# Attention and two mixture layers in one kernel: the stretch between the last expert and the first sorted tile rewritten

## The chip, the cores and the metric

The kernel runs on one core of a Trainium2 chip. The metric is the device time of one execution in microseconds; a lower number is better. TensorE (PE) multiplies, with its weight loads apart (PEld); VectorE (DVE), ScalarE (ACT) and GpSimd (POOL) do elementwise work; SyncE (SP) issues most transfers, and POOL those whose rows are chosen by an index in memory.

## What is computed

The reference is a chain of three stages. The first is attention with hashed buckets; its result, 1536 tokens of 512 numbers, goes through an expert layer in which every expert sees every token, and then through one in which each token goes to one expert:

```python
out = np.zeros((N, D))                       # second stage, N, D, E, F = 1536, 512, 8, 1024
for e in range(E):
    out += P[:, e:e + 1] * (np.maximum(x @ w1[e], 0.0) @ w2[e])
# third stage, on x = out
xn = x / (np.linalg.norm(x, axis=-1, keepdims=True) + 1e-06)
logits = xn @ en.T / tau                     # en: normalised expert_emb
expert_idx = np.argmax(logits, axis=1)
probs = softmax(logits)                      # exp(logits - max) / (sum + 1e-9)
gate_w = probs[np.arange(N), expert_idx]
for e in range(E):
    mask = expert_idx == e
    out[mask] = gate_w[mask, None] * (np.maximum(x[mask] @ w1[e], 0.0) @ w2[e])
```

## The kernel before

Every product in single precision is made of three matmuls on split operands (`matmul_x3`, L444 to L446: low by high, high by high, high by low), so each weight matrix must be split into a high and a low part before use. ACT makes the high parts and DVE the low ones.

**The second stage** goes over 8 experts. An expert works in three groups of 512 tokens, each first up (8 blocks `f`) and then down (8 blocks for 4 token tiles `i` of 128). After each down sum DVE adds the tile to `tok` (L1569). In the last expert, routing of the finished tiles is woven between the matmuls. A token tile `t` (0 to 11) passes these steps: PE turns it (`turn_token`, L793); ACT copies it out as `x_t` (L1091) and takes its sum of squares; PE makes the logits (`token_logits`, L799); DVE chooses the expert (`choose`, L1433 to L1439); PE ranks the tokens (`token_rank`, L804, L805); DVE finds each token's cell (`find_cell`, L1446 to L1463); and PE adds the tile to a table of cells (`table_part`, L811).

**Between the stages** stands the stretch that the change rewrites. Tile 11 is ready only with the very last sum, and passes its steps with nothing beside it. The first sorted tile consists of rows gathered from `x_rows` in memory, where tiles 0 to 9 are stored (an index list, `first_idx`, L1483, a gather by POOL, L585 with `x_row`, and a product with a diagonal matrix `diag`, L939), plus rows of tiles 10 and 11 that are taken from `tok` with a one-hot matrix `hot` (`last_rows`, L838). `HOT` is 10. The sum lies in PSUM banks 2 to 5. ACT and DVE split it into `x_hi` (L1169) and `x_lo` (L1628). Meanwhile DVE makes the inverse norms and the softmax weights of all tokens (L1606 to L1612, with an Exp on ACT at L1197, then L1639 to L1641), and PE and DVE the starts of the experts' tiles (L949, L950, `start_i` at L1618) and the list of rows (L956, L1632 to L1635).

**The third stage** runs over sorted tiles of 128 rows, each with one expert. Each engine goes over the experts' tiles in loops whose bounds it loads from `start_i` (L450, L451). Beside a tile, ACT and DVE split the next expert's weights (L1115 and L1503 for `w2`, L1110 and L1497 for `w1`), and ACT scales the tile before and puts it into `y_row` (L1175), for which it needs the weights `p_now`. POOL's order for a tile is: copy the indices, store `y_row`, gather `p_now` from `weights`, gather the rows of the tile after next. It begins when DVE's weights (`p_ready`) have been stored to memory by SP. SP loads the experts' weights, 2 MB each, in the order written out, as the buffers come free; the load for `w1` of expert 2 waits for the weights' store and for the second gather of rows.

What waits on what is fixed by semaphores and by the order of the code on each engine; nothing is planned at run time but the loop bounds.

## Time and profile before

| | us |
|---|---|
| median of 3 runs | 1612.83 (1612.45 to 1616.38) |
| the profiled execution | 1612.79 |
| its span | 1611.1 |
| PE busy | 1578.6 (98%) |
| DVE busy | 682.7 (42%) |
| ACT busy | 507.7 (32%) |
| POOL busy | 311.4 (19%) |
| granted clock of PE over the span | 0.99 |

The span is the profiled stretch of work; about 1.7 us of the execution's time lie around it. A busy share is an average over all three stages, and the change touches a stretch of about 18 us, so the shares tell little about it. A granted clock of 1.00 means 2.4 GHz, one of 0.50 means 1.2 GHz.

### The profile page before, as it was taken

The page shows a single profiled execution, that of the slowest core. Times are in us where ns is not written, and L with a number is a line of the kernel's source. Part 1 is how long each engine was busy: PE and PEld are TensorE (multiplying, and loading weights), DVE is VectorE, ACT ScalarE, POOL GpSimd, SP SyncE. Part 2 cuts the span into 40 slices and gives each one's busy share as a digit, 9 for nine tenths or more (in the row PEclk, how much of TensorE's full clock was granted, in tenths as well). Part 3 has the DMA queues.
Part 4 walks back from the last instruction along what each step waited for, and adds up shares of the span by engine and source line. Part 5 has one row for each costly group of instructions (what it writes and reads, how often), then busy time and mean ns, then how long its engine had stood idle before and what let it go on. Part 6 is the DMA issues. An engine that isn't in the chain of part 4 may idle for free.

```text
span 1611.1 us, 21916 instructions
## 1 busy us (share of the span) xinstructions
PE 1578.6 (98%) x7637; PEld 1318.6 (82%) x7638; DVE 682.7 (42%) x1237; ACT 507.7 (32%) x933; POOL 311.4 (19%) x522
## 2 busy tenths in 40 slices
PE   7999999999999999999999999999999999899997
PEld 6999998778888888888888888888888887778886
DVE  5888788351211211322221121122232255787666
ACT  4777777211100101211210111021121133476554
POOL 4455443200210120030030021003003000132222
PEclk8999999999999999999999999999999999799999
DMA  6554554100110110110020011011002121574310
GB/s 153 136 128 112 126 121 146 71 1 0 52 53 1 52 52 0 52 52 0 0 100 4 0 52 52 0 52 52 0 0 105 40 79 72 187 291 148 140 46 25
DMA packets 45592, 110.96 MB, mean 69 GB/s; under 512 B 5926, under 2 KB 7974, under 8 KB 45552
## 3 DMA queue, kind: packets, MB, share of 16 engines
q1 hardware_dynamic: 41248, 100.52, 20.1%
q0 software_dynamic: 3504, 8.14, 1.5%
q10 hardware_dynamic: 800, 1.77, 0.5%
q8 instruction: 24, 0.39, 0.1%
q14 instruction: 16, 0.13, 0.0%
HBM read 81.57 MB, written 8.39 MB: 56 GB/s over the span
## 4 chain that ended last, share of the span: by engine, by line
PE 90%; DVE 3%; issue 2%; POOL 2%; DMA 2%; ACT 1%; POOLq 0%; DVEq 0%; ACTq 0%
PE psum L444 25%; PE psum L446 25%; PE psum L445 25%; PE psum L682 3%; PE psum L671 2%; PE psum L695 2%; PE psum L696 1%; PE psum L672 1%; PE psum L653 1%; DVE row_min L1263 1%; PE psum L707 1%; PE psum L971 1%; DVE pt_lo L1253 1%; PE psum L799 1%; DMA x_row<-x_rows,idx_now 1%
## 5 line engine op out<-in xcount | busy, mean ns | idle before, releaser
L1123 ACT ACTIVATE h_hi<-psum 128x512 fp32r<-128x512 f32 x192 | 115.0, 599 | 890.5 <-PE psum L446 890.5
L444 PE MATMUL psum<-xt_lo,w_hi 128*128 128x512 f32 x768 | 305.5, 398 | 0.2 <-DVE xt_lo L1356 0.2
L446 PE MATMUL psum<-xt_hi,w_lo 128*128 128x512 f32 x768 | 304.5, 396 | 0.0
L445 PE MATMUL psum<-xt_hi,w_hi 128*128 128x512 f32 x768 | 304.4, 396 | 0.0
L444 PE MATMUL psum<-w_lo,h_hi 128*128 128x512 f32 x768 | 302.3, 394 | 0.0
L446 PE MATMUL psum<-w_hi,h_lo 128*128 128x512 f32 x768 | 299.3, 390 | 0.0
L445 PE MATMUL psum<-w_hi,h_hi 128*128 128x512 f32 x768 | 299.1, 389 | 0.0
L1514 DVE SCALAR_TENSOR_TENSOR h_lo<-psum,h_hi 128x512 fp32r<-128x512 f32 x192 | 132.8, 692 | 368.5 <-ACT h_hi L1123 368.5
L1569 DVE SCALAR_TENSOR_TENSOR tok<-psum,route,tok 128x512 f32<-128x512 f32 x84 | 57.5, 745 | 355.3 <-PE psum L446 355.3
L477 POOL CAST w_hi<-w_raw 128x512 fp32r<-128x512 f32 x64 | 40.0, 626 | 823.1 <-PE psum L446 813.8
L444 PEld LDWEIGHTS psum<-xt_lo,w_hi 128*128 128x128 f32 x768 | 144.6, 188 | 35.1 <-DVE xt_lo L1356 0.4
L446 PEld LDWEIGHTS psum<-xt_hi,w_lo 128*128 128x128 f32 x768 | 144.6, 188 | 35.1
L445 PEld LDWEIGHTS psum<-xt_hi,w_hi 128*128 128x128 f32 x768 | 144.7, 188 | 34.5
L446 PEld LDWEIGHTS psum<-w_hi,h_lo 128*128 128x128 f32 x768 | 144.1, 188 | 30.4
L444 PEld LDWEIGHTS psum<-w_lo,h_hi 128*128 128x128 f32 x768 | 144.2, 188 | 29.0
L445 PEld LDWEIGHTS psum<-w_hi,h_hi 128*128 128x128 f32 x768 | 144.3, 188 | 28.9
L1253 DVE TENSOR_TENSOR pt_lo<-psum,pt_hi 128x384 fp32r<-128x384 f32 x192 | 98.2, 553 | 35.8 <-ACT pt_hi L1020 34.0
L1027 ACT ACTIVATE prob<-psum,row_bias,row_scale 128x768 f32<-128x768 f32 x96 | 96.6, 1007 | 20.7 <-POOL row_bias L521 20.5
L1020 ACT CAST pt_hi<-psum 128x384 fp32r<-128x384 f32 x192 | 83.3, 487 | 42.4 <-PE psum L682 42.4
L1263 DVE TENSOR_REDUCE row_min<-psum 128x1 f32<-128x768 f32 x96 | 91.1, 949 | 8.7 <-PE psum L672 8.7
L560 POOL TENSOR_TENSOR w_lo<-w_raw,w_hi 128x512 fp32r<-128x512 f32 x64 | 82.7, 1291 | 12.4 <-issue 7.2
L671 PE MATMUL psum<-k_b,q_b 128*128 128x384 f32 x192 | 74.7, 389 | 7.6 <-DMA q_b<-bits 5.0
(264 smaller groups left out, 2026.8 us busy)
## 6 DMA issues: line engine op xcount, KB each, us to landing
w_raw<-in_moe_w_dram SPq DMA_DIRECT2D x25, 2048.0 KB, 8.2
w_raw_odd<-in_moe_w_dram SPq DMA_DIRECT2D x4, 2048.0 KB
k_hh<-k_hi SPq DMA_DIRECT2D x32, 192.0 KB, 3.0
w_raw_even<-in_moe_w_dram SPq DMA_DIRECT2D x3, 2048.0 KB
x_rows<-tok SPq DMA_DIRECT2D x14, 256.0 KB, 2.4
k_raw<-in_k_dram SPq DMA_DIRECT2D x8, 384.0 KB, 3.0
v_raw<-in_v_dram SPq DMA_DIRECT2D x16, 192.0 KB, 3.4
k_b<-k_lo SPq DMA_DIRECT2D x16, 192.0 KB, 3.4
```

What stands on the lines that cost most here:

```text
L444: pe.matmul(acc, a[0], b[1], start=start, stop=False)
L445: pe.matmul(acc, a[0], b[0], start=False, stop=False)
L446: return pe.matmul(acc, a[1], b[0], start=False, stop=stop)
L560: pool.tensor_tensor(w2_s[1][:, f, :], w2_raw[:, f, :], w2_s[0][:, f, :].bitcast(F32), ALU.subtract).then_inc(m1.w2_lo, 1)
L671: pe.matmul(o, q_b[u][:, a], k_b[u][:, b], start=True, stop=False)
L1020: act.copy(pt_hi[half][:, 3 * c:3 * c + 3, a:a + P], psum[:, 4 + c, 0:HALF].rearrange("p (j i) -> p j i", j=3)).then_inc((s_hi_a, s_hi_b)[ ...
L1027: act.activation(prob[t % 2][:].rearrange("p (c j) i -> p c (j i)", c=2), psum[:, 2 * (t % 2):2 * (t % 2) + 2, 0:HALF], ACT.Exp, bias=row_ ...
L1123: act.activation(h_s[0][:, f, :], psum[:, f % 4, :], ACT.Relu).then_inc(m1.h_hi, 1)
L1253: dve.tensor_tensor(pt_lo[half][:, 3 * c:3 * c + 3, a:a + P], psum[:, 4 + c, 0:HALF].rearrange("p (j i) -> p j i", j=3), pt_hi[half][:, 3 ...
L1263: dve.tensor_reduce(row_min[:, c], psum[:, 2 * (t % 2):2 * (t % 2) + 2, 0:HALF], AX.XY, ALU.min).then_inc(s_min, 1)
L1514: dve.scalar_tensor_tensor(h_s[1][:, f, :], psum[:, f % 4, :], 0.0, h_s[0][:, f, :].bitcast(F32), ALU.max, ALU.subtract).then_inc(m1.h_lo, 1)
L1569: dve.scalar_tensor_tensor(tok[:, tile, 0:DM], psum[:, 4 + i, :], route[:, e, tile:tile + 1], tok[:, tile, 0:DM], ALU.mult, ALU.add).then_ ...
```

## The change

Seven things change. (1) The last sum, that of tile 11, is made in two halves of 256 columns, and PE's turn and ACT's copy follow in halves (`turn_half`, `last_token`). (2) The list `first_idx` is asked for one block earlier (`f == 4` for 5), and DVE's split of the last part of `w1` (L1497) moves from before it to behind `choose(10)`. (3) The product with the gathered rows is parted: columns 0 and 1 of four stay ahead of tile 11's logits, 2 and 3 go behind tile 10's last table part, just ahead of tile 11's rows. (4) Inverse norms and softmax sums go from DVE to POOL, but for three reciprocals; the sum of eight is made by three adds. POOL does this between its first and its second gather. (5) ACT takes its Exp behind a wait for the tiles' starts. (6) PE turns the identity four times ahead of tile 11's logits and four times behind the last table part (`keep_busy`). (7) The loop over expert 0's tiles stands ahead of the others with start 0 and an end that ACT and DVE load earlier.

The core of the diff; new semaphores, and the same change of the loop (7) in DVE's part, are left out.

```diff
@@ -609,6 +611,28 @@
         pool.wait_ge(s_x_stored, 16 * HOT)
         pool.wait_ge(s_first_idx, 1)
         gather(x_row[:], x_rows, first_idx[:], s_xrow)
+        squares, inv = per_tok[:, 0, :], per_tok[:, 3, :]
+
+        def row_bc(i):
+            return per_tok[:, i, :].unsqueeze(2).to_broadcast([P, TT, E])
+
+        pool.wait_ge(s_total_in, 1)
+        pool.tensor_tensor(g1[:], logit[:], row_bc(4), ALU.subtract).then_inc(s_p_step, 1)
+        pool.wait_ge(s_norm, 1)
+        pool.tensor_tensor(inv, inv, squares, ALU.mult).then_inc(s_p_step, 1)
+        pool.wait_ge(s_p_step, 2)
+        pool.tensor_tensor(inv, inv, per_tok[:, 2, :], ALU.add).then_inc(s_p_step, 1)
+        pool.wait_ge(s_p_step, 3)
+        pool.tensor_scalar(inv, inv, 0.5, 1e-6, ALU.mult, ALU.add).then_inc(s_p_step, 1)
+        pool.wait_ge(s_norm, 2)
+        pool.tensor_tensor(g1[:], g1[:], row_bc(3), ALU.mult).then_inc(s_act_in, 1)
+        pool.wait_ge(s_act_out, 4)
+        for n in (4, 2):
+            pool.tensor_tensor(g1[:, :, 0:n], g1[:, :, 0:n], g1[:, :, n:2 * n], ALU.add).then_inc(s_p_step, 1)
+            pool.wait_ge(s_p_step, 4 + 4 // n)
+        pool.tensor_tensor(squares, g1[:, :, 0], g1[:, :, 1], ALU.add).then_inc(s_p_step, 1)
+        pool.wait_ge(s_p_step, 7)
+        pool.tensor_scalar(per_tok[:, 1, :], squares, 1e-9, None, ALU.add).then_inc(s_p_sum, 1)
         pool.wait_ge(m2.routed, 1)
         pool.wait_ge(s_x_last, 32)
         pool.wait_ge(s_xrow_t, 1)
@@ -836,14 +860,14 @@
             pe.wait_ge(s_hot, t - HOT + 1)
             for kd in range(KD):
                 mm = pe.matmul(psum[:, 2 + kd, 0:P], tok[:, t, kd * P:(kd + 1) * P], hot[:, t - HOT, :],
-                               start=False, stop=t == TT - 1)
+                               start=t == HOT and kd >= 2, stop=t == TT - 1)
             if t == TT - 1:
                 mm.then_inc(s_xrow_t, 1)
 
         def tokens_between(f, i, n):
 
             t = 2 * CT - 1 + i
-            if t == HOT and f == 5:
+            if t == HOT and f == 4:
                 pe.wait_ge(s_added, 3)
...
@@ -932,23 +956,48 @@
-        turn_token(TT - 1, 0)
-        pe.wait_ge(s_diag, 1)
-        pe.wait_ge(s_xrow, 16)
+
+        def keep_busy(n, bank):
+            for i in range(n):
+                pe.transpose(psum[:, bank, 0:P], ident[:], ident[:])
+
+        def gathered_rows(kds):
+            pe.wait_ge(s_diag, 1)
+            pe.wait_ge(s_xrow, 16)
+            for kd in kds:
+                pe.matmul(psum[:, 2 + kd, 0:P], x_row[:, kd * P:(kd + 1) * P], diag[:], start=kd < 2, stop=False)
+
+        def turn_half(half, bank):
+            for kd in (2 * half, 2 * half + 1):
+                a = kd % 2 * P
+                tr = pe.transpose(psum[:, bank, a:a + P], tok[:, TT - 1, kd * P:kd * P + P], ident[:])
+            return tr
+
+        pe.wait_ge(s_squares, TT - 1)
+        pe.wait_ge(s_tok_half, 1)
+        turn_half(0, 0).then_inc(s_turn_half, 1)
+        pe.wait_ge(m1.y, E * TT + 1)
+        turn_half(1, 7).then_inc(s_turned, 1)
+        gathered_rows((0, 1))
+        keep_busy(4, 5)
         for kd in range(KD):
-            pe.matmul(psum[:, 2 + kd, 0:P], x_row[:, kd * P:(kd + 1) * P], diag[:], start=True, stop=False)
-        token_logits(TT - 1, 1)
+            if kd % 2 == 0:
+                pe.wait_ge(s_copied, TT + kd // 2)
+            mm = pe.matmul(psum[:, 1, 0:E], x_t[:, kd, :], emb_t[:, kd, :], start=(kd == 0), stop=(kd == KD - 1))
+        mm.then_inc(s_logits, 1)
         last_rows(HOT)
         token_rank(TT - 1, 6)
         pe.wait_ge(s_total_in, 1)
         pe.matmul(psum[0:E, 1, 32:33], counts[:, TT % 2, :], ones_b[:, 0:1], start=True, stop=True).then_inc(s_total, 1)
         pe.wait_ge(s_squares, TT)
         table_part(HOT, 0)
+        gathered_rows((2, 3))
         last_rows(TT - 1)
         pe.wait_ge(s_begin_in, 1)
         pe.matmul(psum[0:CELLS, 6, 32:33], earlier[0:E, :], spot[0:E, 5:6], start=True, stop=True)
         pe.matmul(psum[0:1, 6, 48:48 + E + 1], spot[0:E, 4:5], reach[0:E, :], start=True, stop=True).then_inc(s_begin, 1)
         table_part(TT - 1, 0)
+        keep_busy(4, 7)
         pe.wait_ge(s_start, 1)
...
@@ -1091,6 +1140,17 @@
             act.wait_ge(s_copied, t + 1)
             act.activation(psum[:, bank, :], tok[:, t, :], ACT.Square,
+                           accum_out=per_tok[:, 0, t:t + 1]).then_inc(s_squares, 1)
+
+        def last_token():
+            t = TT - 1
+            act.wait_ge(s_logits, t)
+            act.wait_ge(s_turn_half, 1)
+            act.copy(x_t[:, 0:2, :].rearrange("p k i -> p (k i)"), psum[:, 0, 0:256]).then_inc(s_copied, 1)
+            act.wait_ge(s_turned, TT)
+            act.copy(x_t[:, 2:4, :].rearrange("p k i -> p (k i)"), psum[:, 7, 0:256]).then_inc(s_copied, 1)
+            act.wait_ge(s_copied, TT + 1)
+            act.activation(psum[:, 0, :], tok[:, t, :], ACT.Square,
                            accum_out=per_tok[:, 0, t:t + 1]).then_inc(s_squares, 1)
@@ -1193,15 +1252,17 @@
                 w1_hi2(e + 1, w1_raw_of[1 - u])
 
         first_x_hi()
+        act.wait_ge(s_start, 1)
+        first_end = act.value_load(start_i[0:1, 1:2], min_val=1, max_val=SLOTS)
         act.wait_ge(s_act_in, 4)
         act.activation(g1[:], g1[:], ACT.Exp).then_inc(s_act_out, 1)
-        act.wait_ge(s_start, 1)
         act.wait_ge(s_x_lo, 1)
+        tiles2(0, 0, 0, first_end)
         with act.Fori(0, E // 2 - 1) as e2:
-            for u in range(2):
-                expert2(2 * e2 + u, u)
-        expert2(E - 2, 0)
-        expert2(E - 1, 1, more=False)
+            for u in (1, 0):
+                e = 2 * e2 + 2 - u
+                tiles2(e, u, *tile_range(act, e))
+        tiles2(E - 1, 1, *tile_range(act, E - 1), more=False)
...
@@ -1450,6 +1511,8 @@
                                               chosen[:, 0:1].to_broadcast([P, P]), ALU.is_equal, ALU.mult))
                 dve.sem_inc(s_hot, 1)
             if t == TT - 1:
+                dve.wait_ge(s_act_out, 3)
+                dve.reciprocal(per_tok[:, 3, :], per_tok[:, 2, :]).then_inc(s_norm, 1)
                 dve.wait_ge(s_total, 1)
                 link(dve.tensor_scalar(spot[0:E, 6:7], psum[0:E, 1, 32:33], P / 2 - 0.5, EVEN, ALU.add, ALU.add))
                 link(dve.tensor_scalar(spot[0:E, 4:5], spot[0:E, 6:7], EVEN, float(P), ALU.subtract, ALU.max))
@@ -1561,16 +1624,24 @@
                         if i == 0:
                             w1_lo2(0, w1_raw, (0,))
                         choose(2 * CT - 1 + i, 1)
+                        if i == CT - 1:
+                            w1_lo2(0, w1_raw, (KD - 1,))
                         dve.wait_ge(*((s_down_tile, i + 1) if i < CT - 1 else (m1.down, n + 2)))
                     tile = c * CT + i
                     if first:
                         first_y(tile)
                         continue
+                    if last and tile == TT - 1:
+                        for half, done in ((slice(0, 256), s_tok_half), (slice(256, 512), m1.y)):
+                            dve.scalar_tensor_tensor(tok[:, tile, half], psum[:, 4 + i, half], route[:, e, tile:tile + 1],
+                                                     tok[:, tile, half], ALU.mult, ALU.add).then_inc(done, 1)
+                        find_cell(HOT, 6)
+                        continue
                     dve.scalar_tensor_tensor(tok[:, tile, 0:DM], psum[:, 4 + i, :], route[:, e, tile:tile + 1],
                                              tok[:, tile, 0:DM], ALU.mult, ALU.add).then_inc(m1.y, 1)
                     if last and c == CH - 1:
-                        find_cell(2 * CT - 1 + i, 6 if i == CT - 1 else 2)
-                        if i < CT - 1:
+                        find_cell(2 * CT - 1 + i, 2)
+                        if i < CT - 2:
                             w1_lo2(0, w1_raw, (i + 1,))
                         if i == 2:
                             add_part(HOT - 1, 3)
@@ -1601,16 +1672,9 @@
-        dve.wait_ge(s_act_out, 3)
-        root, inv = per_tok[:, 2, :], per_tok[:, 3, :]
-        link(dve.reciprocal(inv, root))
-        link(dve.tensor_tensor(inv, inv, per_tok[:, 0, :], ALU.mult))
-        link(dve.tensor_tensor(inv, inv, root, ALU.add))
-        link(dve.tensor_scalar(inv, inv, 0.5, 1e-6, ALU.mult, ALU.add))
-        link(dve.reciprocal(inv, inv))
-        link(dve.tensor_tensor(g1[:], logit[:], row_bc(4), ALU.subtract))
-        link(dve.tensor_tensor(g1[:], g1[:], row_bc(3), ALU.mult))
-        dve.sem_inc(s_act_in, 1)
+        inv = per_tok[:, 3, :]
+        dve.wait_ge(s_p_step, 4)
+        dve.reciprocal(inv, inv).then_inc(s_norm, 1)
         dve.wait_ge(s_begin, 1)
         link(dve.tensor_copy(begin_col[0:CELLS, :], psum[0:CELLS, 6, 32:33]))
         link(dve.tensor_scalar(slot_of[0:CELLS, :], slot0[0:CELLS, :], begin_col[0:CELLS, 0:1], None, ALU.is_equal))
@@ -1635,9 +1699,8 @@
         link(dve.scalar_tensor_tensor(tab[:, 1:COLS, 0:1], out_at[:, 0:COLS - 1].unsqueeze(2), -1.0,
                                       ids[:, 0:COLS - 1].unsqueeze(2), ALU.add, ALU.add))
         dve.sem_inc(m2.routed, 1)
-        dve.wait_ge(s_act_out, 4)
-        link(dve.tensor_reduce(per_tok[:, 0, :], g1[:], AX.X, ALU.add))
-        link(dve.tensor_scalar(per_tok[:, 1, :], per_tok[:, 0, :], 1e-9, None, ALU.add))
+        first_end = dve.value_load(start_i[0:1, 1:2], min_val=1, max_val=SLOTS)
+        dve.wait_ge(s_p_sum, 1)
         link(dve.reciprocal(per_tok[:, 2, :], per_tok[:, 1, :]))
         dve.sem_inc(s_p_ready, 1)
 
```

**PE from tile 11's turn on.** `tok` turned is L793 before and L973 now; L799 and L986 are the logits of tile 11, L939 and L968 the gathered rows, L838 and L862 the rows of tile 10. Before:

```order
L793 MATMUL psum<-ident,tok 128x128 [waits token_squares,m1_y_added]
L793 MATMUL psum<-ident,tok 128x128 x3
L939 MATMUL psum<-diag,x_row 128x128 [waits x_row_loaded,diag_ready]
L939 MATMUL psum<-diag,x_row 128x128 x3
L799 MATMUL psum<-emb_t,x_t 128x8 [waits token_copied]
L799 MATMUL psum<-emb_t,x_t 128x8 x3
L838 MATMUL psum<-hot,tok 128x128 [waits last_rows_one_hot]
L838 MATMUL psum<-hot,tok 128x128 x3
L804 MATMUL psum<-chosen,prior 128x8 [waits token_chosen]
```

And now:

```order
L973 MATMUL psum<-ident,tok 128x128 [waits last_sum_half,token_squares]
L973 MATMUL psum<-ident,tok 128x128
L973 MATMUL psum<-ident,tok 128x128 [waits m1_y_added]
L973 MATMUL psum<-ident,tok 128x128
L968 MATMUL psum<-diag,x_row 128x128 [waits x_row_loaded,diag_ready]
L968 MATMUL psum<-diag,x_row 128x128
L962 MATMUL psum<-ident 128x128 x4
L986 MATMUL psum<-emb_t,x_t 128x8 [waits token_copied]
L986 MATMUL psum<-emb_t,x_t 128x8
L986 MATMUL psum<-emb_t,x_t 128x8 [waits token_copied]
L986 MATMUL psum<-emb_t,x_t 128x8
L862 MATMUL psum<-hot,tok 128x128 [waits last_rows_one_hot]
```

The turn waits for halves, two of the gathered rows' columns are gone from ahead of the logits, and four turns of the identity stand there.

**PE from tile 10's table part to the first sorted tile.** L811 and L835 are the table part, L949 and L997 the starts, L956 and L1005 the list of rows. Before:

```order
L811 MATMUL psum<-lane_id,cell 96x128 [waits table_added,token_cell,token_squares]
L838 MATMUL psum<-hot,tok 128x128 [waits last_rows_one_hot]
L838 MATMUL psum<-hot,tok 128x128 x3
L949 MATMUL psum<-spot,earlier 96x1 [waits begins_wanted]
L950 MATMUL psum<-reach,spot 1x9
L811 MATMUL psum<-lane_id,cell 96x128 [waits token_cell]
L953 TENSOR_LOAD start_i [waits starts_ready]
L953 ISA x2
L956 MATMUL psum<-slot_of,table 128x21 [waits slots_wanted,table_added]
```

And now:

```order
L835 MATMUL psum<-lane_id,cell 96x128 [waits table_added,token_cell,token_squares]
L968 MATMUL psum<-diag,x_row 128x128 [waits x_row_loaded,diag_ready]
L968 MATMUL psum<-diag,x_row 128x128
L862 MATMUL psum<-hot,tok 128x128 [waits last_rows_one_hot]
L862 MATMUL psum<-hot,tok 128x128 x3
L997 MATMUL psum<-spot,earlier 96x1 [waits begins_wanted]
L998 MATMUL psum<-reach,spot 1x9
L835 MATMUL psum<-lane_id,cell 96x128 [waits token_cell]
L962 MATMUL psum<-ident 128x128 x4
L1002 TENSOR_LOAD start_i [waits starts_ready]
L1002 ISA x2
L1005 MATMUL psum<-slot_of,table 128x21 [waits slots_wanted,table_added]
```

Two columns of the gathered rows now stand between tile 10's table part and tile 11's rows, and four turns of the identity ahead of the load of a bound.

**POOL between its first gather and its loops.** Before:

```order
L585 DMA x_row<-x_rows,first_idx 128x512 [waits first_idx_ready,x_stored]
L585 DMA x_row<-x_rows,tab 128x512 [waits x_row_turned,x_last_stored,m2_routed]
L617 UNCONDITIONAL_BRANCH [waits p_stored]
```

And now:

```order
L587 DMA x_row<-x_rows,first_idx 128x512 [waits first_idx_ready,x_stored]
L620 TENSOR_TENSOR g_61<-logit,per_tok 128x96 [waits totals_wanted]
L622 TENSOR_TENSOR per_tok<-per_tok 128x12 [waits norm_inverse]
L624 TENSOR_TENSOR per_tok<-per_tok 128x12 [waits p_step_pool]
L626 TENSOR_SCALAR per_tok<-per_tok 128x12 [waits p_step_pool]
L628 TENSOR_TENSOR g_61<-g_61,per_tok 128x96 [waits norm_inverse]
L631 TENSOR_TENSOR g_61<-g_61 128x12x4 [waits route_act_out]
L631 TENSOR_TENSOR g_61<-g_61 128x12x2 [waits p_step_pool]
L633 TENSOR_TENSOR per_tok<-g_61 128x12 [waits p_step_pool]
L635 TENSOR_SCALAR per_tok<-per_tok 128x12 [waits p_step_pool]
L587 DMA x_row<-x_rows,tab 128x512 [waits x_row_turned,x_last_stored,m2_routed]
L641 UNCONDITIONAL_BRANCH [waits p_stored]
```

Nine elementwise instructions, each with a wait, stand ahead of the second gather.

## Rows read from the trace of the kernel before

**Rows 1.** Stages: us, busy us of PE, PEld, DVE, ACT, POOL; PEclk, DMA share, GB/s

```profile
1371.00:1376.00 5.00, 3.27 (x16) 1.94 (x16) 3.26 (x15) 0.23 (x1) 1.30 (x1) 0.99 0.22 68
1376.00:1382.00 6.00, 5.93 (x28) 5.68 (x28) 2.60 (x15) 1.29 (x4) 0.00 (x0) 0.50 0.99 289
1382.00:1389.00 7.00, 3.97 (x17) 3.44 (x17) 5.10 (x22) 2.15 (x3) 0.00 (x0) 0.50 0.21 80
1400.00:1410.00 10.00, 10.00 (x48) 8.04 (x48) 9.96 (x14) 8.46 (x14) 2.12 (x3) 1.00 0.85 278
```

**Rows 2.** Timeline of PE, from the last expert to the first sorted tile

```profile
1373.08 0.18 PE L804 MATMUL psum<-chosen,prior 128*128 128x8 bf16 x1 [0.49 <-DVEq L1437]
...
1375.02 0.66 PE L793 MATMUL psum<-ident,tok 128*128 128x128 f32 x4 [0.92 <-DVE tok L1569]
1376.07 2.04 PE L939 MATMUL psum<-diag,x_row 128*128 128x128 f32 x8 [0.40 <-DMA x_row<-x_rows,first_idx]
1377.91 1.71 PE L799 MATMUL psum<-emb_t,x_t 128*128 128x8 f32 x8
1379.48 2.05 PE L838 MATMUL psum<-hot,tok 128*128 128x128 f32 x8
...
1382.46 2.08 PE L838 MATMUL psum<-hot,tok 128*128 128x128 f32 x8 [0.45 <-DVEq L1451]
...
1388.00 0.58 PE L956 MATMUL psum<-slot_of,table 96*128 96x21 f32 x2 [2.58 <-DVEq L1477]
```

**Rows 3.** Timeline of DVE in the same stretch

```profile
1368.39 1.23 DVE L1497 TENSOR_TENSOR w_lo<-w_raw,w_hi 128x1024 fp32r<-128x1024 f32 x1
...
1371.14 0.16 DVE L1483 TENSOR_SCALAR first_idx<-psum 128x1 uint32<-128x1 f32 x1 [1.33 <-PE psum L848]
...
1374.21 0.75 DVE L1569 SCALAR_TENSOR_TENSOR tok<-psum,route,tok 128x512 f32<-128x512 f32 x1 [0.73 <-PE psum L446]
...
1379.66 0.17 DVE L1433 TENSOR_REDUCE per_tok<-psum 128x1 f32<-128x8 f32 x1 [2.39 <-PE psum L799]
...
1381.60 0.17 DVE L1446 TENSOR_TENSOR pick<-psum,chosen 128x8 f32<-128x8 f32 x1 [0.22 <-PE psum L805]
...
1384.38 0.23 DVE L1606 RECIPROCAL per_tok<-per_tok 128x12 f32<-128x12 f32 x1
...
1386.21 0.15 DVE L1615 COPY begin_col<-psum 96x1 f32<-96x1 f32 x1
...
1386.78 0.15 DVE L1618 TENSOR_SCALAR start_i<-psum 1x9 int32<-1x9 f32 x1
```

**Rows 4.** Timeline of ACT, its table load, Exp and two rows of output

```profile
1385.18 1.28 ACT L1197 ACT_TABLE_LOAD   x1
1386.47 0.28 ACT L1197 ACTIVATE g<-g 128x96 f32<-128x96 f32 x1
...
1390.38 0.69 ACT L1175 ACTIVATE y_row<-psum,p_now 128x512 f32<-128x512 f32 x1 [3.62 <-issue]
...
1417.12 0.69 ACT L1175 ACTIVATE y_row<-psum,p_now 128x512 f32<-128x512 f32 x1 [1.86 <-POOLq L607]
```

**Rows 5.** Chain that ended last, pieces by start and length

```profile
1372.28 3.65 DMA x_row<-x_rows,first_idx
...
1390.10 0.24 DVE per_tok L1641
...
1399.86 8.12 DMA x_row<-x_rows,idx_now
```

**Rows 6.** Groups by line and shape, the nearest POOL operation

```profile
L511 POOL TENSOR_TENSOR v_s<-v_raw,v_s 128x384 fp32r<-128x384 f32 x16 | 16.1, 1009 | 1.4
```

**Rows 7.** Timeline of PE at the start of the program

```profile
3.38 4.67 PE L634 MATMUL psum<-ident 128*128 128x128 f32 x24
...
8.07 0.33 PE L653 MATMUL psum<-k_hi,proj_k_lo 128*128 128x384 f32 x1
...
16.32 0.52 PE L672 MATMUL psum<-k_hh,q_t 128*128 128x384 f32 x1
```

More of the change, by code:

```diff
@@ L235, in program @@
     s_p_stored, s_p = sem("p_stored"), sem("p_loaded")
+    s_tok_half, s_turn_half = sem("last_sum_half"), sem("last_turn_half")
+    s_norm, s_p_step, s_p_sum = sem("norm_inverse"), sem("p_step_pool"), sem("p_sum_ready")
     s_diag, s_hot, s_start = sem("diag_ready"), sem("last_rows_one_hot"), sem("starts_ready")
@@ L1147, in expert @@
                     token(2 * CT + 2, 0)
-                    token(2 * CT + 3, 0)
+                    last_token()
             if not last:
@@ L1175, in y_tile, with tiles2 @@
             act.activation(y_row[:], psum[:, 4, :], ACT.Copy, scale=p_now[:, 0:1]).then_inc(s_y2, 1)
-        def expert2(e, u, more=True):
-            first, end = tile_range(act, e)
+        def tiles2(e, u, first, end, more=True):
             with act.Fori(first, end) as i:
@@ L1652, in g_lo, with tiles2 @@
                               ALU.subtract).then_inc(s_g_lo, 1)
-        def expert2(e, u, more=True):
-            first, end = tile_range(dve, e)
+        def tiles2(e, u, first, end, more=True):
             with dve.Fori(first, end) as i:
@@ L1674, in expert2 @@
                 w1_lo2(e + 1, w1_raw_of[1 - u])
+        tiles2(0, 0, 0, first_end)
         with dve.Fori(0, E // 2 - 1) as e2:
-            for u in range(2):
-                expert2(2 * e2 + u, u)
-        expert2(E - 2, 0)
-        expert2(E - 1, 1, more=False)
+            for u in (1, 0):
+                e = 2 * e2 + 2 - u
+                tiles2(e, u, *tile_range(dve, e))
+        tiles2(E - 1, 1, *tile_range(dve, E - 1), more=False)
     block.__exit__(None, None, None)
```

## The prediction

> **What bounds the kernel now.** The table of the profile came first: the profiled execution took 1612.79 us, its span is 1611.1 us and PE is busy for 98% of it. So PE sets the time nearly everywhere, and the change can only bring what PE loses in its stretch. I then read the stages between the last expert and the first sorted tile [rows 1]. In three of them PE has less than its full time, 3.27 of 5.00, 5.93 of 6.00 and 3.97 of 7.00 us, and in two the granted clock is 0.50, which is 1.2 GHz. The 0.99 of the first shows that the clock fell at its very end.
>
> The timelines tell what the path is. PE waits 0.49 us for tile 10's choice, 0.92 us for the last sum and 0.40 us for the first gather [rows 2], which left at 1372.28 and took 3.65 us [rows 5]. Tile 11's logits then stand behind the gathered rows, 1376.07 to 1377.91, and last to 1379.48. Its rank stands behind tile 10's rows, so that DVE picks it up at 1381.60 [rows 2, 3]. I call this moment R. From there DVE is the path: cell, norms and softmax weights, starts. `start_i` is written at 1386.93 (1386.78 and 0.15), which I call T [rows 3]. PE loads a bound, makes the list of rows at 1388.00 and begins the first sorted tile about 0.45 us later, at T + 1.5 [rows 2].
>
> Behind T a second path matters. DVE's weights are ready at 1390.34, T + 3.4; their store and POOL's order for a tile follow, with a gather of rows that takes 8.12 us to land [rows 5], for the 3.65 of the calm one. At 1417.12 ACT had waited 1.86 us for POOL before it could scale a tile [rows 4]. DVE is busy 9.96 of 10.00 us from 1400 to 1410 [rows 1]. So up to the third tile four things are near their limit, and a head start of PE must be matched by POOL and DVE to reach the end.
>
> **The change, part by part.** I make each sum twice: A with the clock at 0.50 from about 1376 as before, B with it at 1.00 as far as T.
>
> *Up to the logits.* `first_idx` is asked for a block earlier and no longer stands behind the split of 1.23 us [rows 3]. An estimate is 1.4 us, by which the first gather lands near 1374.5. Tile 10's choice moves as well, so PE's wait of 0.49 us goes and the last sum starts at 1373.7 for 1374.21. The moved split then lies beside PE's last twelve matmuls or so, and ends about when the last sum can begin; if that cover is gone, it costs up to 1.2 us. Half a sum of 0.75 us, 512 columns, should take between 0.38 and 0.75; I take 0.48, since short operations on DVE cost 0.15 alone [rows 3]. The second turn ends near 1375.1, and the copy of each half lies beside what follows on PE. Then PE does four passes of gathered rows. They cost 0.25 us each at 0.50 (2.04 for eight, [rows 2]) and an estimated 0.13 at 1.00. Four turns of the identity come behind them, 0.19 each (4.67 for 24, [rows 7]) at 0.50, and about half at 1.00. Logits begin at 1376.9 in A and at 1375.9 in B, for 1377.91 before.
>
> *Up to R.* In A the rest is as long as before: R comes 1.0 us earlier. In B the logits take 0.8 for 1.57 us (gain 0.8). Tile 10's rows take half of 2.0, but then tile 11's choice, some 0.95 us on DVE from 1379.66 [rows 3], is what the rank waits for (gain 0.6). R comes 2.0 + 0.8 + 0.6 = 3.4 us earlier.
>
> *From R to T*, 5.33 us before. DVE loses the 1.83 us from 1384.38 to 1386.21 [rows 3] and keeps two reciprocals of 0.23 with their links, so it could take the starts at R + 3.2 for R + 4.6. POOL's chain of three small operations between the reciprocals hides behind DVE's cell. But PE has to deliver the starts, and has four passes of gathered rows more ahead of tile 11's rows. In A these are 1.0 us, half of which the wait of 0.45 us for `hot` covers [rows 2]; the starts come at R + 3.9. In B they come at R + 2.4, and DVE sets R + 3.2. With 0.7 us more for the starts, R to T is 4.6 in A and 3.9 in B. **T comes 1.0 + 0.7 = 1.7 us earlier in A and 3.4 + 1.4 = 4.8 us in B.** The second four turns (0.75 us in A) end before DVE has written T or just behind, and cost nothing up to some 0.4 us. The way from T to the first tile stays 1.5 us.
>
> *What the moved weights cost.* Before, the table load of 1.28 us and the Exp lay ahead of T on ACT [rows 4]. Now ACT first waits for T and loads a bound. Before, two loads and a wait of some 1.3 us for the first tile's low part made up the 3.62 us without work ahead of 1390.38 [rows 4], so one load is about 0.9 (an estimate; between nothing and 1.8). Load, table, Exp: 0.1 + 0.9 + 1.28 + 0.28 = 2.6 us. Then come four operations on POOL of 48 elements and fewer. No row has this shape; 384 elements take 1.009 us [rows 6], which bounds each from above, and nothing is the bound below; I take 0.25 (nearer to the starts' 0.15 on DVE), 0.1 for each wait, 1.4 in all, and then 0.35 for DVE's reciprocal. Weights are ready at T + 4.4 for T + 3.4: **1.0 us of the head start is lost for POOL's path**, with up to 3.0 more at the upper bound. The second gather of rows, which was sent right behind the list, now waits for POOL's sums too, about T + 4.1 for T + 2.9; it lands at T + 7.7, still ahead of PE's turn of it at T + 9.7 (before, 8.2 us after a tile's start), or at T + 8.6 in B.
>
> Exp began right at the load's end, 1386.47 [rows 4], so I count no time between. The Trainium skill, ScalarE: Activation LUTs, "What ACT_TABLE_LOAD costs", gives 1283 ns for the load and some 1380 ns of draining on top. The trace agrees with the first and shows no second; by the page the weights would be 1.4 us later still.
>
> *What the transfers do.* A gather landed in 3.65 us in calm and in 8.12 us beside the 2 MB loads [rows 5]. POOL's gathers fall 1.0 us later relative to DVE, whose progress sends these loads, so they queue behind more of them. Bounds are a gain of 4.5 us (the calm case) and a loss of as much; I take a loss of 0.6. ACT's wait of 1.86 us shows that POOL's path is already on the edge, so this loss passes to PE. DVE enters its loop at T + 4.7 for about T + 5.5 (its weights and two loads), which leaves it 0.8 us in hand and costs nothing.
>
> **Sum.** Gain 1.7 to 4.8 at T, less 1.6. The clock fell after a spell in which PE waited 0.49, 0.92 and 0.40 us. Of these the first goes, the third goes, and four turns are added; it will fall, but later. I take the middle, 3.3 us, and get 3.3 - 1.6 = 1.7 us: 1612.8 - 1.7 = **1611.1 us**. The profiled execution's 1612.79 is the median's 1612.83 but for 0.04, so the sum needs no shift. The loops' new form costs a branch or two that no row shows, bounded by nothing below and by one load's 0.9 above; it is in the 0.9 that ACT saves in its loop's entry.
>
> **Rivals.**
>
> *The clock falls as before* (A). For it: four turns are 0.75 us at most in a stretch of 10, and PE is still without work for some 2 us ahead of the first tile. Against it: the waits before 1376 are 0.9 us shorter and work fills in. Then 1.7 - 1.6 leaves 0.1: 1612.7 us. Turning the identity does raise the clock in this kernel: after 24 turns and hardly anything else, a matmul of 384 columns takes 0.33 us at 8.07, and 0.52 at 16.32 behind a pause [rows 7], so the first ran at the full clock. The Trainium skill, TensorE: Matmul & The Clock Gate, "Part 4: PE-mode transpose", says that transposes don't count as activity for the clock; by it this rival would be certain, and the start of this trace speaks against it. I give it 0.25, my forecast 0.37.
>
> *The clock stays high to T, with the toll as reckoned*: 4.8 - 1.6 = 3.2, 1609.6 us, chance 0.12.
>
> *The clock stays high and the transfers fall well.* If the gather gets ahead of a 2 MB load, it gives back up to 4.5 us and POOL's path is free. Then DVE limits: 4.8 + 0.8 = 5.6, 1607.2 us. For it speaks that the order of gather and load is a matter of a microsecond; against it that POOL is moved to the wrong side. Chance 0.20.
>
> *POOL's path takes over*: its sums hold back the weights and the second gather, and with it SP's load for expert 2, which waits for both. At the upper price (3.0 more) and the full delay of a gather (4.5 for 0.6), the toll is 1.6 + 3.0 + 3.9 = 8.5, and with A's gain of 1.7 the kernel takes 1619.6 us. It turns slower by 0.3% when the toll passes the gain by 4.8, so at 6.5 in A. Against it speaks that nothing on POOL of this size took more than about a third of the upper price. Chance 0.06.
>
> **Numbers.** A measurement of this kernel can tell about 0.3%, 4.8 us, from no change, so the bounds are 1608.0 and 1617.6. Faster: 0.20, the free case. Slower: 0.06. The rest is within. The range goes down to the free case, 1607.0, and up to A with the sums at 0.5 us each on POOL (1.0 more) and a further 0.8 us for the gather, 1614.5; outside are the slower case and a tail of each.
>
> **What would show it.** In the profile after: PE's wait before the last choice gone; logits' start at 1376 to 1377; R at 1378 to 1381; T at 1382 to 1385.3; weights ready at T + 4.4; POOL's nine operations at 0.2 to 0.4 us each; a clock that falls after 1376; ACT's wait for POOL at the third tile longer than 1.86 us. The prediction would be wrong if the clock didn't fall at all, if the gathers land much faster or slower than 8 us, or if PE had slack behind the third tile, which its 98% don't show.

## The result, and the profile after

The changed kernel takes 1616.38 us (median; 1613.83 to 1618.30) and the kernel before, in turns with it on the same chips, 1612.37 (1610.27 to 1617.29). The ratio is 1.0017, with a 95% interval of 1.0010 to 1.0024. So the change costs 2.7 us by the ratio and 4.0 by the medians: less than the 0.3% that the prediction calls "no change", but the forecast was a gain, 1611.1, and its range ended at 1614.5. The profiled execution took 1614.12 us, its span is 1612.4 (1611.1 before). It is one of the 7 shorter of 22 executions (up to 1615.44; the other 15 took 1616.06 to 1618.30), so its trace shows only 1.3 us of the loss.

The way to the first sorted tile did get shorter. These are rows of DVE's timeline of the kernel after, which answer to [rows 3]:

```profile
1369.03 0.16 DVE L1546 TENSOR_SCALAR first_idx<-psum 128x1 uint32<-128x1 f32 x1 [0.58 <-PE psum L872]
...
1371.39 1.23 DVE L1560 TENSOR_TENSOR w_lo<-w_raw,w_hi 128x1024 fp32r<-128x1024 f32 x1
1372.95 0.87 DVE L1636 SCALAR_TENSOR_TENSOR tok<-psum,route,tok 128x256 f32<-128x256 f32 x2 [0.33 <-PE psum L448]
...
1378.35 0.17 DVE L1507 TENSOR_TENSOR pick<-psum,chosen 128x8 f32<-128x8 f32 x1
...
1382.08 0.16 DVE L1682 TENSOR_SCALAR start_i<-psum 1x9 int32<-1x9 f32 x1
```

and rows of PE's timeline, which answer to [rows 2]:

```profile
1375.04 0.96 PE L986 MATMUL psum<-emb_t,x_t 128*128 128x8 f32 x8
...
1377.48 0.18 PE L828 MATMUL psum<-chosen,prior 128*128 128x8 bf16 x1 [0.49 <-DVEq L1498]
...
1383.35 0.37 PE L1005 MATMUL psum<-slot_of,table 96*128 96x21 f32 x2 [1.39 <-DVEq L1540]
1383.76 0.71 PE L446 MATMUL psum<-w_lo,x_hi 128*128 128x512 f32 x1
```

The reader is to see R at 1378.35 (1381.60 before), T at 1382.24 (1386.93 before), and the first sorted tile at 1383.76, T + 1.5 as before. The start is 4.7 us earlier, nearly the 4.8 of case B. Of these, 0.3 are not the change's: ACT's last activation of the second stage, far ahead of the stretch, starts at 1343.36 and started at 1343.67 before.

Some 25 us later all of it is lost. POOL's timeline after:

```profile
1386.05 0.28 POOL L635 TENSOR_SCALAR per_tok<-per_tok 128x12 f32<-128x12 f32 x1
1386.77 1.04 POOL L587 DMA_INDIRECT x_row<-x_rows,tab  x1 [0.45 <-issue]
1390.81 0.19 POOL L479 COPY idx_now<-tab 128x3 uint32 x1 [2.99 <-DMA x_row<-x_rows,tab]
1396.11 1.24 POOL L596 DMA_INDIRECT out_dram<-y_row,idx_now  x1 [5.12 <-issue]
1397.65 1.92 POOL L587 DMA_INDIRECT p_now<-weights,idx_now  x1 [0.31 <-issue]
1399.88 0.95 POOL L587 DMA_INDIRECT x_row<-x_rows,idx_now  x1 [0.30 <-issue]
1407.64 0.19 POOL L479 COPY idx_now<-tab 128x3 uint32 x1 [6.81 <-DMA x_row<-x_rows,idx_now]
```

The same copy of the indices and the same three transfers in POOL's timeline before:

```profile
1395.54 0.69 POOL L477 COPY idx_now<-tab 128x3 uint32 x1 [4.79 <-issue]
1397.24 1.03 POOL L594 DMA_INDIRECT out_dram<-y_row,idx_now  x1 [1.01 <-POOL idx_now L477]
1398.58 0.97 POOL L585 DMA_INDIRECT p_now<-weights,idx_now  x1 [0.31 <-issue]
1399.86 1.47 POOL L585 DMA_INDIRECT x_row<-x_rows,idx_now  x1 [0.30 <-issue]
```

POOL had its indices at 1391.00, 5.2 us earlier than before (1396.23), and stored its first tile only 1.1 us earlier. In front of that store stand 5.12 us in which it waited for nothing that the profile shows ("issue"), for 1.01 before. What queues up behind it shows in ACT's timeline and in the list of PE's waits from 1383 to the end (us in total, times, longest), both after:

```profile
1404.67 0.69 ACT L1235 ACTIVATE y_row<-psum,p_now 128x512 f32<-128x512 f32 x1 [7.10 <-POOLq L609]
```

```profile
PE psum L1020 <- DVE g_row L1709: 5.6, 1, 5.6
PE psum L1005 <- DVEq L1540: 1.4, 1, 1.4
```

ACT lacks the weights' row `p_now` for 7.10 us (1.86 at 1417.12 in [rows 4], a tile later), DVE waits for ACT, PE lacks `g_row` for 5.6 us. And the stages after, in 4 us each, show a second price (columns as in [rows 1]):

```profile
1380.00:1384.00 4.00, 2.11 (x16) 1.59 (x15) 2.97 (x12) 1.17 (x2) 0.60 (x3) 0.98 0.46 173
1384.00:1388.00 4.00, 4.00 (x12) 3.10 (x12) 1.82 (x6) 3.99 (x8) 2.05 (x5) 0.60 0.05 4
...
1404.00:1408.00 4.00, 0.16 (x1) 0.16 (x2) 2.11 (x4) 3.33 (x7) 0.19 (x1) 0.54 1.01 375
1408.00:1412.00 4.00, 4.00 (x16) 3.35 (x17) 2.85 (x5) 2.21 (x5) 2.05 (x2) 0.61 0.52 210
```

PE works 0.16 of 4.00 us, and the granted clock falls to 1.2 GHz again. From 1408 to 1412 it is 0.61 in the mean, which is 0.39 x 4.00 = 1.6 us of work lost.

**What POOL waited for.** The DMA view counts one more kind of packet: "q14 instruction". From 1393 to 1395, after:

```profile
q1 hardware_dynamic: 201, 0.82, 103.0%
q14 instruction: 1, 0.01, 1.0%
```

One packet of 8 KB is fetched from a queue named for instructions, in the midst of SP's 2 MB load for expert 2, which left at 1390.56. Narrower windows put it at 1394.1; POOL's store follows 2.0 us later. Such packets stand in every trace, so what matters is which of them moves. Before has them at 1371.0, 1389.3, 1405.8 and 1407.8 in this stretch, after at 1369.7, 1384.1, 1394.1 and 1408.9. The ones at 1389.3 and 1384.1 come some 2 us behind T in either kernel and are a pair; the one at 1394.1 has moved up from 1405.8 or 1407.8, where POOL was waiting for its gather anyway (6.89 us, until 1408.22). My theory after the result, **F**: the packet is a piece of POOL's own program; the change adds 9 operations and as many waits to POOL's stream and so moves the place at which the next piece is needed; it is now needed when the rings are full of a 2 MB load, and POOL stands still. Its rivals: the **late gather**, that is the toll of the moved sums (the second gather of rows and the weights come too late), and **chance** in how transfers meet.

### The profile page after: what moved, and what is told of

Same layout as the page of the kernel before. It is cut to its first block, busy times and chain, and to the rows that moved or that the text cites. A ratio compares the mean times of both kernels' runs of the same rounds, so it can differ in the third digit from the quotient of the medians.

```text
span 1612.4 us, 21929 instructions
## 1 busy us (share of the span) xinstructions
PE 1576.7 (98%) x7645; PEld 1316.7 (82%) x7646; DVE 680.9 (42%) x1231; ACT 507.8 (31%) x934; POOL 312.7 (19%) x531
## 4 chain that ended last, share of the span: by engine, by line
PE 91%; DVE 3%; issue 2%; POOL 2%; DMA 1%; ACT 1%; DVEq 0%; POOLq 0%; ACTq 0%
PE psum L446 26%; PE psum L448 25%; PE psum L447 25%; PE psum L706 3%; PE psum L695 2%; PE psum L719 2%; PE psum L720 1%; PE psum L696 1%; PE psum L677 1%; DVE row_min L1324 1%; PE psum L731 1%; PE psum L1020 1%; DVE pt_lo L1314 1%; PE psum L823 1%; PE psum L770 0%
## 5 line engine op out<-in xcount | busy, mean ns | idle before, releaser
L706 PE MATMUL psum<-ident,prob 128*128 128x128 f32 x576 | 80.0, 274 | 1.0 <-DVE pt_lo L1314 0.8
```

Of the source, the lines that this page charges most:

```text
L706: tr = pe.transpose(psum[:, 4 + c, j * P:j * P + P], prob[par][:, 3 * c + j, :], ident[:])
```

## The experiments

**1. After, with 24 more instructions on POOL.** They repeat a table at the start of the program (once per instruction, with a wait behind each), almost 1400 us ahead of the place in dispute. No work of the kernel is touched.

```diff
+        for n in range(24):
+            pool.iota(slot_i[:], [[P, COLS]], base=0, channel_multiplier=-P).then_inc(s_pad, 1)
+            pool.wait_ge(s_pad, n + 1)
         pool.iota(slot_i[:], [[P, COLS]], base=0, channel_multiplier=-P).then_inc(s_pool_step, 1)
```

> The changed kernel, with 24 tiny index operations (iota) more on POOL, which repeat the last of its tables while POOL has nothing to do, far ahead of its first gather. Nothing on any path changes but the place of POOL's later instructions in its code. Theory F (a stretch of POOL's code is fetched behind the 2 MB load, and POOL stands still for it at its first output store): the fetch comes 24 instructions earlier, in calm, the 5.1 us ahead of the store shrink to about 1, POOL's gathers go out ahead of the next loads, and the time is 1608 to 1610.5. Theory Q (POOL's path is late by its sums and the Exp behind the starts, and the gathers queue behind the loads whatever the code does): no difference, 1616.

Measured: 1609.08 us (1606.96 to 1612.67), ratio to before 0.9979 (0.9969 to 0.9989). POOL's timeline of this kernel:

```profile
1390.67 0.18 POOL L480 COPY idx_now<-tab 128x3 uint32 x1 [3.04 <-DMA x_row<-x_rows,tab]
1391.87 1.04 POOL L600 DMA_INDIRECT out_dram<-y_row,idx_now  x1 [1.02 <-issue]
1393.21 1.00 POOL L591 DMA_INDIRECT p_now<-weights,idx_now  x1 [0.30 <-issue]
1394.51 1.44 POOL L591 DMA_INDIRECT x_row<-x_rows,idx_now  x1 [0.30 <-issue]
```

The indices are ready as after (1390.85), and the load of 2 MB left as after, at 1390.42; but the store follows the copy of the indices by 1.02 us. The DMA view has no instruction packet from 1388 to 1402, and one at 1370.9 that after does not have. All three transfers have been begun before SP sends its next load at 1395.24. PE's waits from 1383 on:

```profile
PE psum L1009 <- DVEq L1544: 1.4, 1, 1.4
```

The wait of 5.6 us is gone, and 24 instructions more make the kernel 7.3 us faster, as F had it (1608 to 1610.5). POOL's sums and its second gather, at 1386.58, are where they were, so the late gather can't be the cause.

**2. Before, with 9 more.** The edit is the same with `range(9)`, on the kernel before: as many as the change adds.

> The kernel before, with 9 such index operations more on POOL, as many instructions as the change added there. Theory F: the same place of POOL's code is fetched behind the load as in the changed kernel, a stand of 3 to 5 us before the first output store appears, and the time is 1614 to 1618. Theory Q: no difference from before, 1612.4.

Measured: 1621.13 us (1618.49 to 1621.84), ratio 1.0055 (1.0041 to 1.0069). Its POOL timeline and, from 1398 to 1400, its DMA view:

```profile
1395.11 0.47 POOL L478 COPY idx_now<-tab 128x3 uint32 x1 [5.02 <-issue]
1400.82 1.03 POOL L598 DMA_INDIRECT out_dram<-y_row,idx_now  x1 [5.24 <-issue]
1402.16 1.91 POOL L589 DMA_INDIRECT p_now<-weights,idx_now  x1 [0.31 <-issue]
```

```profile
q14 instruction: 1, 0.01, 1.0%
```

Nine instructions of no use, at the start of POOL's program, cost this kernel 9 us at its 1400th: the same stand of 5.2 us at the same store, with the packet at 1398.8, 2.0 us ahead of it. PE waits 5.1 us for `g_row`. F had the mechanism, but the loss is larger than expected (1614 to 1618), and this trace, of 1618.49 us, shows some 6 of the 9 us.

**3. After, with the second gather ahead of POOL's four sums.** If the late gather is the cause, this should help.

```diff
+        pool.wait_ge(m2.routed, 1)
+        pool.wait_ge(s_x_last, 32)
+        pool.wait_ge(s_xrow_t, 1)
+        gather(x_row[:], x_rows, tab[:, 1, 1:2], s_xrow)
         pool.wait_ge(s_act_out, 4)
...
-        pool.wait_ge(m2.routed, 1)
-        pool.wait_ge(s_x_last, 32)
-        pool.wait_ge(s_xrow_t, 1)
-        gather(x_row[:], x_rows, tab[:, 1, 1:2], s_xrow)
```

> The changed kernel with the second gather of rows put ahead of POOL's four sums. Theory F: the count of instructions ahead of the first output store is the same, the stand stays or grows, since the 2 MB load behind this gather starts earlier; 1615 to 1618. Theory Q: this gather and what hangs on it come some 1 to 2 us earlier, 1613 to 1615.

Measured: 1619.05 us (1618.94 to 1620.26), ratio 1.0043 (1.0028 to 1.0058). POOL's timeline:

```profile
1391.85 0.19 POOL L479 COPY idx_now<-tab 128x3 uint32 x1 [4.15 <-issue]
1398.07 3.65 POOL L596 DMA_INDIRECT out_dram<-y_row,idx_now  x1 [6.03 <-issue]
```

The gather leaves at 1385.40 (1386.77 after), but so does SP's load, 1388.88 for 1390.56, and the instruction packet comes at 1396.0. The stand grows to 6.0 us, the store's own issue takes 3.65, ACT waits 10.2 us. That is above both expectations, 1613 to 1615 and 1615 to 1618. It isn't a clean test of the late gather: with it, the weights' store falls back to 1388.04 (1386.67 after), and POOL's indices are ready 1.0 us later than after, not earlier. It fits F in that an earlier load ahead of the packet goes with a longer stand.

**4. After, with inverse norms and softmax weights back on DVE** (part 4 of the change undone: the 9 operations leave POOL, reduce and two adds return to DVE).

> The changed kernel with inverse norms and softmax weights back on DVE; POOL has none of its nine operations, and Exp stays behind the starts on ACT. Theory F: no stand at the first output store; the starts come 1.2 to 1.8 us later than in the changed kernel; 1609 to 1611. Theory Q: the weights are ready 0.5 us earlier relative to the starts and 1 us later in all; 1615 to 1617.

Measured: 1609.84 us (1608.67 to 1611.19), ratio 0.9984 (0.9975 to 0.9993). The store is at 1395.29 with 1.01 us ahead of it. POOL's stream is as long as before, and the stand is gone (F: 1609 to 1611). The packets are placed as before, at 1387.2, 1405.3 and 1407.1. This alone doesn't tell F from the late gather; with kernels 1 and 2 it does, since they keep every sum where it was.

**5 and 8. Kernel 1 without `keep_busy`, and kernel 1 with the last sum whole.** With the stand away, do two other parts of the change pay?

```diff
-        keep_busy(4, 5)
...
-        keep_busy(4, 7)
```

```diff
-                        for half, done in ((slice(0, 256), s_tok_half), (slice(256, 512), m1.y)):
-                            dve.scalar_tensor_tensor(tok[:, tile, half], psum[:, 4 + i, half], route[:, e, tile:tile + 1],
-                                                     tok[:, tile, half], ALU.mult, ALU.add).then_inc(done, 1)
+                        dve.scalar_tensor_tensor(tok[:, tile, 0:DM], psum[:, 4 + i, :], route[:, e, tile:tile + 1],
+                                                 tok[:, tile, 0:DM], ALU.mult, ALU.add).then_inc(m1.y, 1)
```

> The changed kernel with the 24 index operations of e1_after_24_more and without the eight turns of the identity. Theory F says nothing on them. If the turns hold the clock: it falls between 1376 and 1381, the starts come 1 to 3 us later than in e1, and the time is 1610 to 1612. If they don't count as activity: the clock falls at about 1384 as in e1, and the time is e1's 1609.1 or up to 0.7 less for the work left out.

> As e1_after_24_more, with the last sum made whole (one operation of 512 columns); PE's turn and ACT's copy are still in two parts. By my sum the first turn starts 0.3 us later and the whole path shifts by 0.2 to 0.4 us: 1609.3 to 1609.5, which can't be told from e1's 1609.1; DVE's operation takes 0.75 us for the 0.87 of the two halves.

Measured: 1608.38 us (1606.50 to 1609.66), ratio 0.9972 (0.9961 to 0.9983), and 1608.56 us (1607.82 to 1610.87), ratio 0.9978 (0.9967 to 0.9988). Kernel 1 has 0.9979. Neither part brings anything that can be measured; a whole sum was expected to cost 0.2 to 0.4 us, which these runs can't tell. Without the turns the clock is 1.00 to past 1384 as well:

```profile
1380.00:1384.00 4.00, 2.37 (x18) 1.79 (x17) 2.95 (x15) 0.72 (x2) 1.01 (x5) 1.00 0.90 339
1384.00:1388.00 4.00, 3.00 (x8) 2.45 (x9) 1.72 (x7) 2.94 (x5) 1.00 (x4) 0.67 0.01 2
```

**6. Kernel 1 with ACT's Exp ahead of its wait for the starts** (part 5 undone; `act.wait_ge(s_start, 1)` and the load of `first_end` go behind the Exp).

> As e1_after_24_more, with ACT's Exp ahead of its wait for the starts, as it was before the change. Theory F with the toll of my prediction (POOL's path 1.0 us late relative to the starts, since the table load of 1.28 us and a load of a bound lie behind them): weights and second gather come about 2 us earlier, and the time is 1607 to 1608.5. Theory Q in its weak form (with the fetch gone, POOL's path no longer sets anything): 1609.1 as e1.

Measured: 1608.71 us (1606.97 to 1615.32), ratio 0.9984 (0.9971 to 0.9996), just above the expected 1608.5, but in two groups, nine executions at 1607 to 1611 and three at 1615.2 to 1615.3. The profiled execution is of the second (1615.32). Its POOL and SP timelines:

```profile
1394.29 5.39 POOL L591 DMA_INDIRECT p_now<-weights,idx_now  x1 [0.30 <-issue]
```

```profile
1394.37 0.38 SPq L440 DMA_DIRECT2D w_raw<-in_moe_w_dram  x1
```

POOL begins its gather 0.08 us ahead of SP's 2 MB load and is held for 5.39 us, for 1.00 in kernel 1; PE waits 7.1 us. That is a second way to the same loss, with no instruction packet in it. What holds POOL there is not shown. That the load is sent at the same moment isn't enough: in the kernel after and in kernel 2 POOL's gather of rows begins within 0.01 us of a load of 2 MB (1399.88 and 1399.87; 1404.37 and 1404.38), and takes 0.95 us. The kernel before has executions of 1616 to 1618 now and then, whose profile I don't have; that they are of this kind is a guess.

**7. Before, with 33 more.** The control for kernel 1: is it the change that gains, or the 24?

> The kernel before with 33 index operations more on POOL: the 9 of e2_before_9_more and 24 more. Theory F: the fetch comes early, in calm, no stand at the output store, 1612.3 as before. If instead the operations themselves, not the place of the code, made e2 slow: 1621 or more.

Measured: 1611.93 us (1610.74 to 1616.87), ratio 0.9999 (0.9987 to 1.0011). The store at 1395.81 has 1.01 us ahead of it. One packet has gone from the stretch (left behind T are 1387.9 and 1406.5) and stands at 1243.3 instead, where POOL has nothing to do. Before was in a good place already, so more instructions bring it nothing, and kernel 1's gain over it is the change's.

**9 and 10. The best of these, and SP kept behind POOL.** Kernel 6 without `keep_busy`, where SP in addition waits for a semaphore before its load of expert 3's `w2`: for POOL's first store and gather of `p_now` to land (9, `s_y_free`), or for the third gather of rows (10, `s_xrow`). The edit of 10:

```diff
             sp.wait_ge(m2.w2_lo, KF * (split_until + 1))
+            if e == 3:
+                sp.wait_ge(s_xrow, 48)
```

> As e5_no_turns (24 index operations, no turns), with Exp ahead of the starts as in e6, and with SP's 2 MB load of w2 for expert 3 held back until POOL's first pair of store and gather of p_now has landed. e6 showed POOL's gather of p_now taking 5.39 us when this load was issued at the same moment, 0.08 us apart, in the runs at 1615. Theory F extended (POOL stands wherever its own small transfers or descriptors meet a 2 MB load): both the stand and the slow runs go, 1605.5 to 1608. Rival: holding the load back makes it late for ACT at the fourth tile, 1609 or more.

> As e9_load_after_weights_row, but the load waits until the gather of rows behind it has landed as well. If the gather then lands in about 4 us for 8, the load is sent at about 1397, 2 us later than in e1, and the time is 1605 to 1607.5; if the load becomes late, more than e9's.

Measured: 1608.35 us (1607.41 to 1609.08), ratio 0.9974 (0.9965 to 0.9983), and 1608.16 us (1607.45 to 1609.05), ratio 0.9976 (0.9966 to 0.9986). In kernel 9 the load leaves at 1397.12, and POOL's gather of `p_now` is short:

```profile
1394.33 1.00 POOL L593 DMA_INDIRECT p_now<-weights,idx_now  x1 [0.30 <-issue]
```

None of their 19 executions is in the late group of kernel 6 (3 of 12); since these kernels lack the turns as well, and the group is small, that the wait removed it is likely and not shown. Both are slower than expected (1605.5 to 1608 and 1605 to 1607.5). They beat both given kernels, by some 4 and 8 us; between them and kernels 1, 5 and 8 the runs tell nothing apart.

**11. After, unpadded, with SP's load for expert 2 held back.** The packet stays where the change put it, and the load is taken away from in front of it.

```diff
         sp.wait_ge(m2.w1_lo, KD)
+        sp.wait_ge(s_y_free, 2)
         sp.wait_ge(m2.w1_in, 32)
         sp.dma_start(w1_raw_of[0][:], m2.wa[2]).then_inc(m2.w1_in, 16)
```

> The changed kernel with its code as it is, and SP's first 2 MB load of the stage (w1 for expert 2) held back until POOL's first store and gather have landed. Theory F: the fetch is still needed at the same place, but has no load ahead of it; the 5.1 us ahead of the store shrink to 1 to 2.5, the next load is not delayed by more than 5 us, and the time is 1607 to 1611. If the stand of POOL has nothing to do with the load, it stays at about 5 us and the time at 1616 or more.

Measured: 1612.75 us (1610.82 to 1614.43), ratio 1.0005 (0.9997 to 1.0014). POOL's and SP's timelines:

```profile
1391.69 0.19 POOL L480 COPY idx_now<-tab 128x3 uint32 x1 [2.94 <-DMA x_row<-x_rows,tab]
1394.72 1.19 POOL L597 DMA_INDIRECT out_dram<-y_row,idx_now  x1 [2.85 <-issue]
1396.22 1.98 POOL L588 DMA_INDIRECT p_now<-weights,idx_now  x1 [0.30 <-issue]
```

```profile
1399.88 0.37 SPq L433 DMA_DIRECT2D w_raw<-in_moe_w_dram  x1
```

Now nothing large is in the rings, and the packet is at 1392.8, 0.9 us behind the copy of the indices (3.1 us behind it after). The stand is 2.85 us: 1.8 over the 1.02 of a kernel that needs no packet, where the load made it 4.1 over. So by these two traces the fetch alone costs 1.8 us and the queueing behind the load 2.3 more. This way 3.6 of the 7.3 us come back, less than expected (1607 to 1611, with a stand of 1 to 2.5). The rest I put down to a load that is now 9 us late: PE waits for `w_lo`, for rows and for `g_row` by 0.2 to 1.3 us at a time between 1404 and 1420, and the windows show it busy 2.74 of 4.00 us from 1404 on.

## Why the prediction was wrong

**Where it was right.** The steps up to the starts: PE's waits for tile 10's choice and for the first gather gone; R within its window (1378 to 1381); T at 1382.24 (1382 to 1385.3); T + 1.5 to the first tile. The moved weights: POOL's operations took 0.20 to 0.38 us each, and DVE's last reciprocal ended at 1386.59, T + 4.35, where T + 4.4 was forecast. Exp began at 1384.71, right at the end of the table load (1383.42 + 1.28); so the further 1.4 us by the Trainium skill, ScalarE: Activation LUTs, "What ACT_TABLE_LOAD costs", did not show here either. Two details missed: the logits began at 1375.04, a microsecond ahead of the sign given for them (1376 to 1377), since the last sum started at 1372.95 and not at 1373.7; and tile 11's rank, which case B had waiting for its choice, did so for 0.49 us at 1377.48, so the logits' lead was gone again at R.

**The gain at T: right mechanism, wrong size.** I took 3.3, the middle of 1.7 and 4.8, since "it will fall, but later". The clock fell only at the first sorted tile (windows above: 0.98 up to 1384), and T came 4.7 us earlier. The reason given for it, that turns of the identity help, is not borne out: without them (kernel 5) the time is the same. But single traces differ. Kernels 9 and 10, without turns too, have a granted clock of 0.50 all through 1380 to 1388, and kernel 2, with nothing of the change, has 1.00 up to 1380 and 0.75 up to 1384 where before has 0.50. The windows of kernels 10 and 2:

```profile
1380.00:1384.00 4.00, 2.52 (x14) 2.07 (x13) 2.70 (x12) 2.15 (x3) 0.95 (x5) 0.50 0.54 205
```

```profile
1380.00:1384.00 4.00, 2.83 (x15) 2.33 (x14) 2.84 (x15) 0.46 (x2) 0.00 (x0) 0.75 0.90 343
```

So neither the turns nor the change fix by themselves when the clock falls, and how much of the 4.7 is the clock's isn't separated. Whether transposes count for the clock, which the Trainium skill, TensorE: Matmul & The Clock Gate, "Part 4: PE-mode transpose", denies, this place doesn't settle.

**The step that failed** is "What the transfers do", where it says "I take a loss of 0.6": it counts how a gather queues behind loads, and has no term for POOL itself standing still in front of its store. The toll behind T, 1.6 in the sum, was 4.7 + 4.0 = 8.7 us by the medians (4.7 + 1.3 = 6.0 by the two traces). With the instruction packet moved away, in kernel 1, 7.3 us of it are gone by the medians and 7.1 between the profiled executions (1614.12 and 1607.00). Their parts are in these two traces: 5.6 us of PE's wait and 1.6 us of work lost at the lower clock behind it, 7.2 in all.

How large the toll is without the stand stays open. By the medians kernel 1 gains 1612.37 - 1609.08 = 3.3 us, which leaves 4.7 - 3.3 = 1.4, near the 1.6 of the sum and the rival "the clock stays high to T, with the toll as reckoned" (1609.6 us, chance 0.12). But its profiled execution gains 1612.79 - 1607.00 = 5.8, more than the 4.7 at T, as if nothing were lost there, which is the rival at 1607.2. Its executions spread from 1606.96 to 1612.67, so that the 1.4 comes so near the 1.6 can be luck.

**Why no rival covered it.** The slower one had the right place, POOL's path, and even the size of the toll (8.5 us). But its mechanism was the price of the sums and the slow landing of a gather, both of which were near the forecast (T + 4.35 for T + 4.4; a gather of rows from 1399.88 landed at 1407.6, some 7.8 us), and it was joined to the small gain of A. F is another: 9 operations more in a stream, an 8 KB packet that is needed at another moment, and a 2 MB load in front of it. Shown is: instructions without work bring the stand (kernel 2) and take it away (kernel 1); an instruction packet is some 2 us ahead of the late store in the four kernels that have the stand with or without a load in front (after, 2, 3, 11: 1394.1, 1398.8, 1396.0, 1392.8) while in before, 1, 4 and 7 the last one ahead of the store is some 8 us away; less load ahead shortens the stand (11). The late gather falls with kernel 1, and chance with the intervals of 1 and 2. That the packet holds POOL's own code, and not another engine's, is inferred from that it moves with POOL's instructions: one packet of before's at 1405.8 or 1407.8 stands at 1398.8 with 9 more and at 1243.3 with 33 more, and after's of 1394.1 stands at 1370.9 with 24 more, while the others stay within 4 us of their places. The trace names only its queue.

**Open.** Which of the change's parts makes the net 3.3 us. Not the turns and not the halves (5, 8), and hardly POOL's sums (kernel 4 keeps 0.9984 without them; its interval meets kernel 1's). Left are the earlier list, the parted rows and the loop's form, which weren't tried one by one. Open too is what the longer executions of the changed kernel lose, whose median is 2.7 us further from before's than the profiled ones are apart.

## What to carry to other kernels

A change can be right in nearly all its steps and lose by where it puts the rest of an engine's program: when an engine shows "issue" of several us in front of a DMA instruction, look for an instruction packet in the DMA view at that time, and test with instructions that do nothing. Before you judge a change of a few us on an engine whose stream it makes longer or shorter, run it at two or three lengths of that stream, and run the kernel before at as many: here the one went from 1616.4 to 1609.1 and the other from 1612.4 to 1621.1. And where a small transfer that others wait for is held in some executions beside a 2 MB load, try a wait on the loading queue: here it cost nothing that the runs can tell (1608.35 and 1608.16 for 1608.71), and the late executions did not come back.
